# An attention block ahead of two MLPs: the softmax spread over three engines in 480-column operations, keys read in place, the block sums of v by matmul, and the first MLP begun with its first half of the tokens

## What is computed

```python
block, window = (32, 16)
k_sum = k.reshape(B, H, nb, block, D).max(axis=3)      # nb = 24 blocks
v_sum = v.reshape(B, H, nb, block, D).mean(axis=3)
scores_l = scale * q @ k.T, kept where |i - j| < window
scores_s = scale * q @ k_sum.T + log(block)
a = softmax(concatenate([scores_l, scores_s]))          # divided by sum + 1e-9
x = a @ concatenate([v, v_sum])                         # as 1536 tokens x 512
xn = x / sqrt(mean(x*x) + 1e-6) * rms_g
h = silu(xn @ w_gate) * (xn @ w_val)                    # 512 -> 1536
x2 = h @ w_out                                          # 1536 -> 512
h2 = x2 @ w_in;  out = (h2 - tanh(h2)) @ w_out2         # 512 -> 2048 -> 512
```

## Time and profile before

| what | value |
|---|---|
| median of 3 runs | 694.68 us (694.16 to 695.09) |
| span of the profiled execution | 692.5 us |
| PE busy | 648.3 us, 94% |
| DVE busy | 331.9 us, 48% |
| ACT busy | 271.8 us, 39% |
| POOL busy | 31.9 us, 5% |
| transfers | 53.34 MB, mean 77 GB/s |
| mean granted clock of PE | 0.975 |

### The profile page before, as it was taken

How to read it: one execution, slowest core, us unless ns; L and a number is a source line. 1 busy time by engine, 2 the same in 40 slices (tenths; PEclk the granted TensorE clock), 3 DMA queues, 4 the chain that set the end, 5 groups by cost and what they waited for, 6 DMA issues and landing times.

```text
span 692.5 us, 11670 instructions
## 1 busy us (share of the span) xinstructions
PE 648.3 (94%) x4176; PEld 606.3 (88%) x4176; DVE 331.9 (48%) x754; ACT 271.8 (39%) x677; POOL 31.9 (5%) x66
## 2 busy tenths in 40 slices
PE   7273699999999999999999999999999999999997
PEld 7162589999999999999989999999999999989886
DVE  2573775676675323444444445555521254444442
ACT  3184554556454223333333333333311143333332
POOL 2012410001100000000000000000000000000000
PEclk9598799999999999999999999999999999999999
DMA  7674723313431212222222242222203022122202
GB/s 157 139 151 130 180 62 79 75 49 95 98 90 41 61 54 69 72 69 68 65 61 61 61 137 62 67 73 72 76 24 99 1 65 71 62 61 61 61 15 91
DMA packets 105852, 53.34 MB, mean 77 GB/s; under 512 B 46560, under 2 KB 99808, under 8 KB 105440
## 3 DMA queue, kind: packets, MB, share of 16 engines
q1 hardware_dynamic: 104096, 49.82, 27.4%
q10 hardware_dynamic: 1728, 3.15, 1.2%
HBM read 49.81 MB, written 3.15 MB: 76 GB/s over the span
## 4 chain that ended last, share of the span: by engine, by line
PE 85%; DMA 6%; DVE 3%; ACT 2%; SPq 1%; issue 1%; POOL 1%; DVEq 0%; ACTq 0%; POOLq 0%
PE bank L543 20%; PE bank L545 20%; PE bank L544 20%; PE bank L636 6%; PE bank L637 6%; PE bank L635 6%; DMA blk<-in_v_dram 6%; PE bank L521 1%; PE bank L500 1%; SPq L228 1%; ACT xT_hi L817 1%; ACT pr_b L799 1%; POOL blk L388 1%; DVE xT_lo L1056 1%; PE bank L485 1%
## 5 line engine op out<-in xcount | busy, mean ns | idle before, releaser
L543 PE MATMUL bank<-xT_hi,x_hi 128*128 128x384 f32 x448 | 151.6, 338 | 0.6 <-DVE xT_lo L1056 0.6
L545 PE MATMUL bank<-xT_hi,x_lo 128*128 128x384 f32 x448 | 150.2, 335 | 0.0
L544 PE MATMUL bank<-xT_lo,x_hi 128*128 128x384 f32 x448 | 150.2, 335 | 0.0
L1063 DVE TENSOR_TENSOR h_lo<-pd,h_hi 128x384 fp32r<-128x384 f32 (+1 forms) x112 | 62.9, 561 | 70.4 <-ACT h_hi L872 37.1
L543 PEld LDWEIGHTS bank<-xT_hi,x_hi 128*128 128x128 f32 x448 | 84.1, 188 | 3.3 <-DVE xT_lo L1056 0.9
L544 PEld LDWEIGHTS bank<-xT_lo,x_hi 128*128 128x128 f32 x448 | 84.1, 188 | 1.4
L545 PEld LDWEIGHTS bank<-xT_hi,x_lo 128*128 128x128 f32 x448 | 84.1, 188 | 0.0
L637 PE MATMUL bank<-y_hi,h_lo 128*128 128x512 f32 x192 | 76.0, 396 | 0.0
L636 PE MATMUL bank<-y_lo,h_hi 128*128 128x512 f32 x192 | 76.0, 396 | 0.0
L635 PE MATMUL bank<-y_hi,h_hi 128*128 128x512 f32 x192 | 75.9, 395 | 0.0
L1063 DVE TENSOR_TENSOR y_lo<-y_raw,y_hi 128x512 fp32r<-128x512 f32 x56 | 38.5, 688 | 77.3 <-ACT y_hi L832 77.3
(11 more groups left out here) (102 smaller groups left out, 903.6 us busy)
## 6 DMA issues: line engine op xcount, KB each, us to landing
x_raw<-in_moe_w_in_dram SPq DMA_DIRECT2D x32, 256.0 KB, 3.0
y_raw<-in_moe_w_out_dram SPq DMA_DIRECT2D x32, 256.0 KB, 2.7
x_raw<-in_moe_w_gate_dram SPq DMA_DIRECT2D x24, 256.0 KB, 3.0
y_raw<-in_moe_w_val_dram SPq DMA_DIRECT2D x24, 256.0 KB, 3.3
z_raw<-in_moe_w_out_dram SPq DMA_DIRECT2D x16, 384.0 KB, 3.4
kn<-in_k_dram SPq DMA_DIRECT2D x12, 256.0 KB, 5.1
blk<-in_v_dram SPq DMA_DIRECT2D x4, 768.0 KB
out_dram<-stage ACTq DMA_DIRECT2D x12, 256.0 KB, 2.5
```

The lines of the kernel that those rows point to most:

```text
L543: nc.tensor.matmul(dst, w_hi, a_hi, start=start, stop=False)
L544: nc.tensor.matmul(dst, w_hi, a_lo, start=False, stop=False)
L545: return nc.tensor.matmul(dst, w_lo, a_hi, start=False, stop=stop)
L1063: nc.vector.tensor_tensor(dst, full, high.bitcast(f32), ALU.subtract).then_inc(done, 1)
```

## The change

- Batch 0's keys are loaded with six neighbouring rows of a head on each partition (`k_rows`, pieces of 1,536 bytes), DVE puts them in order (`arrange_k`), and PE transposes them so that ACT's copy writes them back in position (`copy_rows`). Batch 0's v is loaded in the same way (`v_rows`), and PE makes its block sums by six matmuls with a 0/1 matrix `ind` (`block_sums`), so batch 0 loads no `blk`. Batch 1 keeps `blk` and POOL's halvings, all five now after batch 0's last `inverse_rms`.
- The window of keys is read in place from `kT` (16 products of 96 columns), and the 24 block maxima are eight products of their own. No `kwin` is copied.
- `shift` is, for each of the two halves of the heads (par 0 and 1), one 480-column add of the mask and one maximum on DVE; POOL subtracts the maximum (`centre`), ACT takes one 480-column exponential. The sum of the weights comes out of `weigh_values` through a 65th column of ones in v. ACT, not DVE, copies the transposed weights.
- `rms_g` is multiplied in `scale_x` (with a broadcast copy `g_bc`), so `xT_high` and `xT_low` are one operation each, no longer four.
- The first pair of group 0 does both columns' b=0 halves before the b=1 halves; batch 1's keys and queries are all transposed in that pair (queries by DVE's `copy_q1`). The attention tile woven with pair i is now tile 5+i, and tile 11 lies in `down_first`. Loops are written out.

The core of the diff:

```diff
+            def centre(T, par):
+                u = 2 * T + par
+                pool.wait_ge(maxed, u + 1)
+                nc.gpsimd.tensor_tensor(sm[u % 4][:], sm[u % 4][:],
+                                        mx[:, u % 4, :].unsqueeze(2).to_broadcast([P, PAIRS, KEYS]),
+                                        ALU.subtract).then_inc(centred, 1)
...
+            for T in range(TPB):
+                centre(T, 0)
+                centre(T, 1)
...
+                if T >= 2:
+                    inverse_rms(T - 2)
...
+            inverse_rms(TPB - 2)
+            inverse_rms(TPB - 1)
+            pool.wait_ge(blk_in, 32)
+            for level in range(1, LEVELS + 1):
+                add_halves(level)
...
+            def block_sums():
+                pe.wait_ge(v_rows_in, 16)
+                pe.wait_ge(ind_done, 1)
+                for r in range(ROWS):
+                    last = nc.tensor.matmul(out_bank(1)[WIN:KEYS, :], ind[:, r, :], v_rows[:, :, r * D:(r + 1) * D],
+                                            start=r == 0, stop=r == ROWS - 1)
+                last.then_inc(means_mm, 1)
...
+            keep_clock_up(30)
+            for c in range(PAIRS):
+                transpose_k(c)
+                if c < PAIRS - 1:
+                    keep_clock_up(2)
+            transpose_q(0)
+            transpose_q(1)
+            scores(0)
+            block_sums()
+            transpose_q(2)
+            for T in range(TPB):
+                transpose_probs(T, 0)
+                if T + 1 < TPB:
+                    scores(T + 1)
+                if 3 + T < TPB:
+                    transpose_q(3 + T)
+                if T >= 1:
+                    weigh_values(T - 1, 1)
+                if T >= 2:
+                    transpose_x(T - 2)
+                transpose_probs(T, 1)
+                weigh_values(T, 0)
...
+            for i in range(1, J1 // 2):
+                T = TPB + i - 1
+                gate(0, 2 * i, 0)
+                scores(T)
+                val(0, 2 * i, 0)
+                gate(0, 2 * i, 1)
+                val(0, 2 * i, 1)
+                if T > TPB:
+                    transpose_x(T - 1)
+                gate(0, 2 * i + 1, 0)
+                transpose_probs(T, 0)
+                val(0, 2 * i + 1, 0)
+                weigh_values(T, 0)
+                gate(0, 2 * i + 1, 1)
+                transpose_probs(T, 1)
+                val(0, 2 * i + 1, 1)
+                weigh_values(T, 1)
...
+            for T in range(1, TPB):
+                copy_probs(T, 0)
+                if 3 + T < TPB:
+                    copy_q(3 + T)
+                if T + 1 < TPB:
+                    exp(T + 1, 0)
+                if T >= 2:
+                    xT_high(T - 2)
+                square(T - 1)
+                copy_probs(T, 1)
+                if T + 1 < TPB:
+                    exp(T + 1, 1)
...
+            for T in range(1, TPB):
+                normalise(T - 1)
+                if T + 1 < TPB:
+                    shift(T + 1, 0)
+                    shift(T + 1, 1)
+                if T >= 2:
+                    xT_low(T - 2)
+                scale_x(T - 1)
+                if T == TPB - 2:
+                    split_x(0)
+                    split_y(0)
+            normalise(TPB - 1)
```

More of the change, by code:

```diff
@@ L165, in attention_then_two_mlps @@
+        vw_late_in = [sem(f"vw_late_in{i}") for i in range(2)]
         x_in = [sem(f"x_in{i}") for i in range(2)]
@@ L732, in _ @@
+            T = NT - 1
+            scores(T)
+            down_first(0, 0)
+            transpose_x(T - 1)
+            transpose_probs(T, 0)
+            down_first(0, 1)
+            weigh_values(T, 0)
+            transpose_probs(T, 1)
+            down_first(0, 2)
+            weigh_values(T, 1)
+            down_first(0, 3)
+            transpose_x(T)
             for g in range(G):
                 if g:
-                    for s in range(2):
-                        up_first(g, 0, s)
-                    with pe.Fori(1, J1 // 2) as i:
-                        for s in range(2):
-                            up_first(g, i, s)
@@ L751, in _ @@
-                down_second(g, J2 // 2 - 1, 1, final=True)
+                    for i in range(J1 // 2):
+                        for j, b in halves(g, i):
+                            gate(g, j, b)
+                            val(g, j, b)
+                    for d in range(KC):
+                        down_first(g, d)
+                up_second(g, 0)
+                for j in range(1, J2):
+                    up_second(g, j)
+                    down_second(g, j - 1)
+                down_second(g, J2 - 1)
@@ new lines, in _ @@
+            square(TPB - 1)
+            xT_high(TPB - 2)
+            tanh_half(0, 0, 0)
+            split_y(1)
+            high_h(0, 0, 0)
+            xT_high(TPB - 1)
+            tanh_half(0, 1, 0)
+            copy_k1(0)
+            high_h(0, 1, 0)
+            for r in range(1, 4):
+                copy_k1(r)
+            tanh_half(0, 0, 1)
+            copy_k1(4)
+            high_h(0, 0, 1)
+            copy_k1(5)
+            tanh_half(0, 1, 1)
+            split_x(2)
+            high_h(0, 1, 1)
@@ L952, in _ @@
+            T = NT - 1
+            square(T - 1)
+            exp(T, 0)
+            exp(T, 1)
+            for d in range(KC):
+                if d == 1:
+                    xT_high(T - 1)
+                    copy_probs(T, 0)
+                if d == 2:
+                    copy_probs(T, 1)
+                if d == 3:
+                    square(T)
+                split_z(2 * d + 2)
+                x2_high(0, d)
+                split_z(2 * d + 3)
+            xT_high(T)
             for g in range(G):
@@ new lines, in _ @@
+            xT_low(TPB - 2)
+            split_x(1)
+            scale_x(TPB - 1)
+            split_y(1)
+            gated(0, 0, 0)
+            product(0, 0, 0)
+            xT_low(TPB - 1)
+            low_h(0, 0, 0)
+            half(0, 1, 0)
+            for r in range(2):
+                copy_q1(r)
+            half(0, 0, 1)
+            for r in range(2, 5):
+                copy_q1(r)
+            dve.wait_ge(k1_copied, ROWS)
+            for c in range(2):
+                block_maxima(1, c)
```

1489 lines of the change are left out of this document (689 added, 800 removed).

## The result

The changed kernel takes **733.97 us** (median of 4 runs, 731.38 to 737.67), the kernel before 694.85 in the same session: ratio **1.057**, 95% interval 1.054 to 1.060. It is slower, by 39 us; I had predicted 710 with a range of 691 to 723. The sign and the way were right, the size was not. The profiled execution took 731.38 us with a span of 729.6.

The account below looks back on a forecast made before the run. PE bounds the kernel, busy 648.3 of 692.5 us. down_first: 68.4 + 29.2 + 127.6 + 4.1 + 5 = 234.3 against 218.3, +16.0, span 708.5; plus 2.2 to the median, rounded to 710, range 691 to 723.

Parts of the forecast that it names:

- The sign and the way: Whole kernel: slower by over 0.2%, chance 0.78, with PE's waits on the scaled x in the pairs as main step.
- What goes: Batch 0: PE's waits for q and the scaled x, both behind blk transfers, disappear, a gain of about 29 us.
- the second wait: Batch 0: PE's 14.8 us for the scaled x, because POOL's first halving waits for blk; forecast to go.
- The start: Start of batch 0: first scores at about 15.8 us, block_sums taking 5.3 and ending at 22.4.
- Scores 1.3: A tile's scores on PE: 1.3 us, against 1.05 before, with 24 narrow products in place of 16.
- The period of 8.0: Batch 0: 8.0 us per tile, from one division to the next through DVE, POOL and ACT, against 5.4 before.
- The pairs' wait 5.25: Four pairs: PE idles 5.25 us each at transpose_x, as DVE's scaling stands behind product and low part.
- The 4 us on `x_lo`: Ahead of the second pair: PE waits some 4 us for x_lo, which stands late in DVE's stream.
- DVE beside POOL 5: First pair's halvings and each tile's centre: DVE and POOL hold each other up, 5 us in all, bounds 1 and 12.
- The 2.66: Evidence for DVE held up by POOL: a scaling beside a halving took 2.66 us instead of 0.48.
- PE's clock falls in batch 0: Rival, batch 0: PE idles 3.3 us per period and its work runs at half clock, +15 us, 725; chance 0.09.
- tile 11's 4.1: Tile 11, ahead of or in down_first: adds 4.1 us for scores, weights, values and x.

Follow-up runs that it names:

- before_halvings_late: The kernel before, with only POOL's halvings of batch 1's value rows moved behind batch 0's last inverse_rms: 691.94 us, ratio 0.9955.
- fill_batch0: The changed kernel with 14 identity matmuls on PE ahead of transpose_probs(T, 0) for tiles 1 to 5 in batch 0: 725.75 us, ratio 1.044.
- pairs_order: The changed kernel with both shifts, then scale_x, earlier in DVE's order in the pairs, and POOL's inverse root ahead of its subtractions: 706.32 us, ratio 1.016.
- fill_pairs_20: The changed kernel with 20 identity matmuls on PE in each of the four waits at transpose_x: 725.19 us, ratio 1.043.
- scale_early: The changed kernel with DVE's scale_x(T - 1) ahead of half(0, j, 1) in the four pairs, instead of behind it: 722.06 us, ratio 1.040.

## Why the prediction was wrong in size, step by step

- **What goes**: right. No wait for `blk` or q is left. But the 14.8 us of the second wait were not all there to be gained: `before_halvings_late` got 5.9 us at the first gate, as SyncE's late windows stood behind it.
- **The start**: scores at 17.47 for 15.8; `block_sums` 5.33 for 5.3, its end at 24.6 for 22.4. 1.7 of the 2.2 were in the start.
- **Scores 1.3**: wrong. 32 wide and 16 narrow matmul instructions take 1.8 us at the full clock (25.58 to 27.40); the narrow ones cost some 0.07 each, which I hadn't priced apart. For tile 0 and in the five pairs nothing hides it: 0.5 and 2.6 us.
- **The period of 8.0**: the size right at the full clock (7.9 in `fill_batch0`), 9.2 as it ran; the chain that sets it was the other one, through PE. My terms add up to 8.14, and POOL's `centre` took 0.99 for the 1.2 in them.
- **The pairs' wait 5.25**: right, 5.05, four times, at the named place and for the named reason (`pairs_order`). The 4 us on `x_lo`: right. **DVE beside POOL 5**: about right (3.9 to some 5.7 in the pair, 5.9 in the median), and by the named mechanism. The 2.66 that I had set beside it was a scaling with one wide input; the low part at 4.40, with two, is the clean case.
- **The step that failed**: "PE's clock falls in batch 0", which I made a rival of 0.09 and only in batch 0. I priced it at 15 there; it cost about 7. It belonged in the sum, at every wait that I had just forecast. The row was there: the clock at 0.50 at 18 us while PE waited from 15.1. I forecast four waits of 5.25 us in the pairs and priced the gates behind them at the full clock. "Each period has five groups of PE work" was the argument against it; in the trace one wait of 2.6 us in a tile was followed by the half level.

The missed 20.7 us at `down_first`, from what the runs showed. In batch 0, 9.7: start 1.7, tile 0's scores 0.5, clock 6.9 (from tile 1's scores to the first gate 52.5 us, in `fill_batch0` 45.7), and 0.6 that no run separated. In the pairs, 10.9: clock 8.2 at the four waits (`fill_pairs_20`), clock again some 2.2 behind the 4.24 us for `x_lo` (1.9 in its gate, 0.4 in the scores), scores 2.6 (five tiles), 0.2 unseparated, and 2.3 to the other side, since of tile 11's 4.1 only the scores' 1.8 stand ahead of `down_first`. So the clock is 17 of the 20.7. The median adds 2.6 more to the error, since this profile's execution, 731.4, was the fastest of the four.

## What to carry to other kernels

A forecast wait of TensorE must be priced twice, as idle time and as the work behind it at half clock: here 5.05 us cost 7.1 as a mean, and 3.31 still cost the clock three times in four. Where an engine's order is written by hand, put each instruction at the moment when its input is ready, not beside the work it belongs to: three such moves (shift, scale, inverse root) were worth 28 us with no instruction less. And a wait may cover another one behind it, or the work that is moved may get in the way elsewhere: removing 14.8 us gave 3. So the length of a wait alone doesn't say what removing it gives, in either direction.

## What the runs showed of the hardware

- The granted clock fell at a wait of only 2.6 us in batch 0 (PE idle to 31.75, clock 1.0 in the window at 31, 0.50 in that at 32), between small groups of short matmuls, and took more than 5 us of PE work to return in the pair shown. The same wait doesn't always have the same price: of four waits of 3.31 us in `scale_early`, behind the same work, three were followed by the half level and one was not. I had taken it for a matter of long waits.
- The Trainium skill (SBUF — State Buffer, Who interferes with whom) has a DVE operation with two SBUF inputs and a POOL operation that reads SBUF block each other for the whole instruction. The trace agrees: 4.40 us for a low part beside a halving of some 4.5. I had not expected the other side: POOL's small `msq`, which reads four bytes a partition, took 0.75 us instead of 0.19 beside a low part (147.69 in the changed kernel, 80.74 with DVE idle).
- A DMA issue on SyncE, 1.0 us at 66.03, took 10.9 at 49.82 in `before_halvings_late`: an issue in a queue can itself be the long piece of a chain.
